# Moving a decay tile, a factor tile and the gate rows from the serial start into the woven first block, with other PSUM banks for the first two state updates

## The reference, cut to what matters

```python
for t in range(S):                                   # layer 1, per head
    m_new = maximum(f[t] + m, i[t])
    f_stab, i_stab = exp(f[t] + m - m_new), exp(i[t] - m_new)
    C = f_stab * C + i_stab * outer(v[t], k[t]);  n = f_stab * n + i_stab * k[t]
    y[t] = sigmoid(o[t]) * (C @ q[t]) / maximum(abs(n @ q[t]), 1.0)
x = (sigmoid(x @ w_gate) * (x @ w_val)) @ w_out      # layer 2
xn = x / sqrt(mean(x * x) + 1e-6) * rms_g            # layer 3
out = (silu(xn @ w_gate2) * (xn @ w_val2)) @ w_out2
```

## Time and profile before

| | us |
|---|---|
| median of 3 runs | 479.87 (479.75 to 481.87) |
| the profiled execution | 479.75 |
| its span | 478.0 |
| PE busy | 471.9 |
| DVE, ACT, POOL busy | 235.6, 196.1, 102.8 |

### The profile page before, as it was taken

The page is one execution under the profiler, slowest core; times in us unless marked ns, Lnnn a source line. Parts: engine busy times, 40 slices in busy tenths (PEclk is TensorE's granted clock), DMA queues, the critical chain, the costliest instruction groups (busy, mean ns, idle before and its releaser), DMA issues.

```text
span 478.0 us, 9965 instructions
## 1 busy us (share of the span) xinstructions
PE 471.9 (99%) x4115; PEld 455.8 (95%) x4115; DVE 235.6 (49%) x515; ACT 196.1 (41%) x404; POOL 102.8 (22%) x142
## 2 busy tenths in 40 slices
PE   8999999999999999999999999999999999999997
PEld 3899989999999999999999999999999999999997
DVE  8858944562766265435434525560455045504550
ACT  4778346623461636153415744330233023302330
POOL 4989910111111110100004968000000000000000
PEclk9899999999999999999999999999999999999999
DMA  7674610111122011100241520001000100010001
GB/s 259 208 242 136 186 46 29 60 45 45 32 85 60 1 45 57 46 1 1 100 149 31 193 93 1 2 1 39 5 1 2 41 1 3 0 43 1 2 2 41
DMA packets 11475, 27.92 MB, mean 58 GB/s; under 512 B 1526, under 2 KB 5830, under 8 KB 11430
## 3 DMA queue, kind: packets, MB, share of 16 engines
q1 hardware_dynamic: 11110, 27.20, 17.7%
q10 hardware_dynamic: 320, 0.08, 0.1%
HBM read 25.23 MB, written 1.97 MB: 57 GB/s over the span
## 4 chain that ended last, share of the span: by engine, by line
PE 89%; DVE 4%; ACT 2%; POOL 1%; DMA 1%; issue 1%; DVEq 0%; ACTq 0%; POOLq 0%
PE bank L1010 26%; PE bank L961 9%; PE bank L962 9%; PE bank L1030 9%; PE bank L1031 9%; PE bank L1032 8%; PE bank L964 6%; PE bank L909 3%; PE bank L882 2%; PE bank L1040 2%; PE bank L837 2%; PE bank L901 1%; DMA raw_x<-in_w_gv 1%; PE bank L858 1%; PE bank L860 1%
## 5 line engine op out<-in xcount | busy, mean ns | idle before, releaser
L961 PE MATMUL bank<-x_hi,wgv_hi 128*128 128x256 f32 x432 | 121.1, 290 | 0.0
L962 PE MATMUL bank<-x_lo,wgv_hi 128*128 128x256 f32 x432 | 118.0, 283 | 0.0
L585 ACT ACTIVATE sg<-bank 128x256 f32<-128x256 f32 (+1 forms) x120 | 51.2, 427 | 156.5 <-PE bank L962 79.6
L1030 PE MATMUL bank<-wo_hi,h_hi 128*128 128x320 f32 x288 | 90.3, 314 | 0.7 <-DVE h_lo L797 0.7
L792 DVE TENSOR_TENSOR hf<-sg,bank 128x256 f32<-128x256 f32 (+1 forms) x120 | 56.7, 473 | 67.0 <-ACT sg L585 64.1
L1010 PE MATMUL bank<-x_hi,wgv_hi 64*128 64x384 f32 x576 | 89.0, 333 | 0.0
L1031 PE MATMUL bank<-wo_lo,h_hi 128*128 128x320 f32 x288 | 89.0, 309 | 0.0
L1032 PE MATMUL bank<-wo_hi,h_lo 128*128 128x320 f32 x288 | 89.0, 309 | 0.0
L961 PEld LDWEIGHTS bank<-x_hi,wgv_hi 128*128 128x128 f32 x432 | 82.6, 191 | 1.3
L962 PEld LDWEIGHTS bank<-x_lo,wgv_hi 128*128 128x128 f32 x432 | 82.7, 191 | 0.4
L964 PE MATMUL bank<-x_hi,wgv_lo 128*128 128x256 f32 x288 | 81.4, 283 | 0.0
(11 more groups left out here) (116 smaller groups left out, 522.1 us busy)
## 6 DMA issues: line engine op xcount, KB each, us to landing
step<-in_w_gv SPq DMA_DIRECT2D x7, 576.0 KB, 3.8
step<-in_vok SPq DMA_DIRECT2D x12, 324.0 KB, 3.0
step<-in_qk_t SPq DMA_DIRECT2D x24, 160.0 KB
raw_x<-in_w_gv SPq DMA_DIRECT2D x5, 576.0 KB, 4.8
raw_p<-in_w_gv SPq DMA_DIRECT2D x4, 576.0 KB, 4.9
y<-y_tok SPq DMA_DIRECT2D x12, 160.0 KB, 1.8
step<-in_vok SPq DMA_DIRECT2D x10, 180.0 KB, 3.5
step<-in_q_t SPq DMA_DIRECT2D x10, 180.0 KB, 2.6
```

The costliest lines, as they stand in the source:

```text
L585: act.activation(sg[:, f % 2, 0:w], g_view(lay, n), ACT.Sigmoid).then_inc(sg_done, 1)
L961: pe.matmul(ps, wgv_hi[:, wc, s, cs], x_hi[:, xs, s, :], start=(s == 0), stop=False)
L962: mm = pe.matmul(ps, wgv_hi[:, wc, s, cs], x_lo[:, xs, s, :], start=False, stop=(s == 2))
L1030: pe.matmul(ps, h[0][:, f, ts], wo_hi[:, f, :], start=(f == 0), stop=False)
```

## The change

1. **The table FIRST.** The PE, ACT, POOL and DVE pieces of tile 2 and 3 stand two slots later than before (S2 in slot 3 instead of 1, K2 and N2 in 5 instead of 3, D3 in 7 instead of 5, S3 and T2 in 9 instead of 7, K3 and N3 in 11, Y3 in 12), T3 in 14 instead of 12, F2 in 14 and R2 in 15. D2 and R1 are no longer part of the serial start: they stand in slots 1 and 2. The gate rows of part 2 are spread over slots 4, 10, 12 and 13.
2. **Banks.** The state updates of tiles 0 and 1 go to PSUM banks 7 and 5 instead of 3 and 1. `hidden(0, 1)` no longer waits for `cn_done`; D2 waits for `cn_done` 2 and R1 for `cn_done` 1.
3. **The serial start.** On DVE, the steps 3 and 4 of the rows of part 1 stand behind the tiles' T and K. On POOL, `vk` of tiles 0 and 1 and the split of chunk 0 stand ahead of the `l_row` step of part 1, and the wait for `consts` 3 is gone. On ACT, F1 stands behind the copies of chunks 1 and 2.
4. **d_rhs.** POOL sets all of it (128x2048) to zero ahead of the first `consts`; DVE and ACT then fill 48 rows each instead of 64. `l_row` has 48 rows instead of 64; `half_neg` is set later.

```diff
-FIRST = [[], [("S", 2)], [], [("K", 2), ("N", 2)], [("Y", 2)], [("D", 3)], [], [("S", 3), ("T", 2)], [("A", 2, 0)],
-         [("K", 3), ("N", 3)], [("Y", 3), ("A", 2, 1)], [("A", 2, 2)], [("T", 3), ("A", 2, 3), ("A", 2, 4)], [("F", 2)],
-         [("R", 2)], []]
+FIRST = [[], [("D", 2)], [("R", 1)], [("S", 2)], [("A", 2, 0)], [("K", 2), ("N", 2)], [("Y", 2)], [("D", 3)],
+         [], [("S", 3), ("T", 2)], [("A", 2, 1)], [("K", 3), ("N", 3)], [("Y", 3), ("A", 2, 2)], [("A", 2, 3), ("A", 2, 4)],
+         [("T", 3), ("F", 2)], [("R", 2)]]
...
-            return bank[(3, 1)[n]] if n < 2 else bank[4]
+            return bank[(7, 5)[n]] if n < 2 else bank[4]
...
-            pool.memset(half_neg[:, :], -0.5).then_inc(consts, 1)
+            pool.memset(d_rhs[:, :, :].bitcast(F32), 0.0).then_inc(consts, 1)
...
-            pool.wait_ge(consts, 3)
+            piece(("D", 0))
+            piece(("D", 1))
+            split(0, 0)
...
-            piece(("D", 0))
-            piece(("D", 1))
-            for c in range(4):
+            for c in range(1, 4):
                 split(0, c)
-            piece(("D", 2))
...
-            piece(("F", 1))
             high(0, 1)
             high(0, 2)
+            piece(("F", 1))
             piece(("T", 0))
             piece(("T", 1))
-            piece(("D", 2))
-            piece(("R", 1))
             high(0, 3)
...
-            for sub in range(5):
-                rows(1, sub)
+            rows(1, 0)
+            rows(1, 1)
+            rows(1, 2)
...
             for n in range(B):
                 piece(("T", n))
+            rows(1, 3)
             for n in range(B):
                 piece(("K", n))
+            rows(1, 4)
...
-                        if n > B:
-                            pe.wait_ge(cn_done, min(n, NT - B))
+                        pe.wait_ge(cn_done, min(n, NT - B))
...
-                if n == 1:
-
-                    pe.wait_ge(cn_done, B)
...
-            piece(("D", 2))
-            piece(("R", 1))
```

More of the change, by code:

```diff
@@ L132, in mlstm_moe_kernel @@
         d_lhs = sb("d_lhs", [P, S], F32R)
-        l_row = sb("l_row", [2 * Q, S], F32R)
+        l_row = sb("l_row", [Q + R, S], F32R)
         cst = [sb(f"cst{b}", [KR, HE], F32) for b in range(B)]
@@ L460, in _ @@
                                         pattern=[[D, nh], [0, D1]], channel_multiplier=-1))
+            pool.memset(half_neg[:, :], -0.5)
             pool.memset(eps[:, :], EPS).then_inc(consts, 1)
-            pool.wait_ge(consts, 3)
+            piece(("D", 0))
+            piece(("D", 1))
+            split(0, 0)
             pool.wait_ge(high_done, 2)
@@ L562, in _ @@
             for b in range(B):
-                act.activation(d_rhs[2 * Q:P, H * b:H * b + H, :],
-                               sel[2 * Q:P, b, :].unsqueeze(2).to_broadcast([2 * Q, H, P]),
+                act.activation(d_rhs[2 * Q:3 * Q + R, H * b:H * b + H, :],
+                               sel[2 * Q:3 * Q + R, b, :].unsqueeze(2).to_broadcast([Q + R, H, P]),
                                ACT.Copy).then_inc(selc_done, 1)
@@ L766, in _ @@
             for b in range(B):
-                dve.tensor_tensor(d_rhs[0:2 * Q, H * b:H * b + H, :],
-                                  l_row[:, 0:P].bitcast(F32).unsqueeze(1).to_broadcast([2 * Q, H, P]),
-                                  sel[0:2 * Q, b, :].unsqueeze(2).to_broadcast([2 * Q, H, P]), ALU.mult).then_inc(drhs_done, 1)
-            for sub in range(5):
-                rows(1, sub)
+                dve.tensor_tensor(d_rhs[0:Q + R, H * b:H * b + H, :],
+                                  l_row[:, 0:P].bitcast(F32).unsqueeze(1).to_broadcast([Q + R, H, P]),
+                                  sel[0:Q + R, b, :].unsqueeze(2).to_broadcast([Q + R, H, P]), ALU.mult).then_inc(drhs_done, 1)
+            rows(1, 0)
+            rows(1, 1)
+            rows(1, 2)
             for n in range(B):
@@ L866, in piece @@
                     pe.wait_ge(lend_done, n)
+                    pe.wait_ge(cn_done, 1)
                     if n > 1:
```

## The result

| | before | with the change |
|---|---|---|
| median, us | 479.87 (5 runs, 479.75 to 481.87) | 484.55 (5 runs, 483.95 to 485.38) |
| ratio to before | | 1.0088, 95% interval 1.0064 to 1.011 |
| profiled execution, us | 479.75 | 484.59 |
| its span, us | 478.0 | 482.8 |

The account below looks back on a forecast made before the run. The prediction took PE, busy 471.9 of 478.0 us, as the bound. Its terms, -1.6 - 0.25 + 1.4 + 0.9 = +0.45 on the profiled 479.75, gave 480.2 us, with a range from 478.7 to 482.0.

Parts of the forecast that it names:

- The gaps of slots 12 and 13, -1.6: PE's idle of 0.88 and 0.70 us waiting for DVE in slots 12 and 13 would go: -1.6 us.
- D2 and R1 between the blocks, +1.4: On PE, D2 and R1 leave a gap and stand between hidden blocks, all on the path: +1.4 us.
- The wait at K2, +0.9: PE would wait at K2 until 37.5 us for ACT's chain with four table loads and DVE's weighing: +0.9 us.
- A table switch with a drain: Rival: on ACT, a pause behind each of four table loads ahead of K2, 5.2 us more, 485.4 us; chance 0.01.
- The start, -0.25: PE would start `hidden(0, 0)` at 22.2 us, as DVE's last copy of Y1 ends earlier: -0.25 us.
- The memset of `d_rhs`, hidden: POOL's memset would delay the constants by 1.8 us, covered by 2.9 us before PE's first D: no cost.
- DVE steps 3 and 4 of part 1, nothing won: These steps, 0.6 us, leave a place where DVE then waited for PE: no gain.
- The clock as a rival: Clock falls after idle ahead of `hidden(0, 0)` or at K2; 3.4 us of hidden blocks lose 1.7: 481.9 us; chance 0.13.

Follow-up runs that it names:

- run 7: Kernel before with only Y3 and the rows of part 2 moved behind the last `h_lo`, T3, F2 and R2 later: 478.82 us, ratio 0.9962.
- run 1: Changed kernel with POOL's `l_row` step back ahead of `vk` of tiles 0 and 1 and the split of chunk 0: 480.58 us, ratio 1.0003.
- run 6: Changed kernel with POOL's order of before, no memset of `d_rhs`, and R1 in slot 1 behind D2: 479.39 us, ratio 0.998.
- run 3: Kernel before with only POOL's `vk` of tiles 0 and 1 and split of chunk 0 put ahead of `l_row`: 484.5 us, ratio 1.0059.
- run 4: Changed kernel with nine more matmuls on zeros on PE between S1 and N0: 484.33 us, ratio 1.007.
- run 5: Changed kernel with POOL's order of before and without the memset of `d_rhs`: 481.95 us, ratio 1.0025.

## Why the prediction was wrong, step by step

- **The gaps of slots 12 and 13, -1.6: right.** No idle in the changed kernel; run 7 measured this part alone at -1.8 us (0.9962 of 480.77, with an interval from -0.8 to -2.8), close to the 1.6 of the two waits.
- **D2 and R1 between the blocks, +1.4: right.** D2 took 30.67 to 31.59 us, R1 about 0.4.
- **The wait at K2, +0.9: right** in mechanism and size, 0.84 in the changed kernel and 0.85 in run 1. K2 was forecast 15.3 us behind the first hidden block and came 15.4 behind it. Run 6 showed the cause, the table loads.
- **A table switch with a drain: fell.** The Sigmoid began 0.01 to 0.02 us behind its load each time, as in the earlier trace rows.
- **The start, -0.25: this step failed.** It came out at +4.28. The prediction weighed POOL's new order only for DVE's last copy in Y1, 9 us later, and priced the moved POOL pieces nowhere else. It had the means to see it: POOL idles for 5 us behind the constants before, DVE is busy all that time, and the prediction itself read from the earlier trace rows that a DVE copy took 0.88 beside a POOL step and might end 0.6 earlier without it. It did not ask what DVE does at 10.8 us, where the order let `vk` start. In its place the runs showed this: `vk` and the first split hold up three DVE steps, the weighing starts 1.6 us later, PE idles 2.0 us ahead of N0, and 10.3 us run at the low clock. Run 1 takes the whole loss away with this one part; run 3 brings 0.6% with it alone.
- **The memset of `d_rhs`, hidden: only nearly.** Its 1.8 us was right (2.44 to 4.24), and the first D on PE was not later for it. But the masks of `bdm` now ran until 10.3 us, in the time of DVE's gate rows and fill, which the prediction did not ask about; DVE's fill began 0.28 later, and PE waited 0.3 for `d_rhs` ahead of 8.63 (0.2 in run 6, without the memset and with D at 8.30).
- **"DVE steps 3 and 4 of part 1, nothing won": right**, but they were the only reserve, 0.55 us, against 2.1 us of delay (three steps of 0.52, 0.58 and 0.70, and 0.3 by which the fill of `d_rhs` began later).
- **The clock as a rival** was priced at one more stretch of 3.4 us in the hidden blocks, 1.7 us. It came as 10.3 us in the serial start, where 3.4 had been before. N0 and N1 alone lost 2.9 us by it. With 1.63 for the late N0 this makes 4.6; 0.3 came back, since T1 no longer waited for Y1. The step had the sign right and the place wrong: it looked at idle that the table made, not at idle in the serial start.

How much of the 4.3 us is lateness and how much the clock is told by the profile (1.6 and 2.9) but not by a run of its own: run 4, made for it, moved the low clock instead of taking it away. One comparison on record bears on it: at the same mean clock of 0.989 the changed kernel took 484.0 to 484.6 us and the kernel before 481.8 to 482.3. So some 2.5 us of the loss stay when both have the low clock for equally long, and some 2.2 are what the kernel before itself loses between 0.996 and 0.989. Why the low clock lasts longer in the changed kernel stays open.

## What to carry to other kernels

A wait that seems useless on an engine with nothing to do can keep it out of another engine's way: before a POOL step is let go earlier, read what DVE does at that time, and remember that one profile shows one phase of several. Where two engines disturb each other, add the delay on the one that the next stage waits for, and look whether the idle that it makes on PE comes where the clock can fall. And try the parts of a bundle apart: here the late Y3 alone won 0.4% (run 7), POOL's order alone lost 0.6% (run 3), and the rest cost about what the late Y3 won (run 1, with both: 1.0003).

## What the runs showed of the hardware

- **DVE beside POOL.** A scan of 16 rows went from 0.41 to 0.93 us, a cast of 16x128 from 0.22 to 0.92, each ending just behind a POOL step that it did not depend on. POOL suffers too: a select of 0.31 took 1.17 beside DVE's fill of `d_rhs`. The Trainium skill (SBUF — State Buffer, section "SBUF: two separate sides") has DVE and GpSimd take turns on a shared port pair for whole instructions. By that rule, the trace agrees: the scan was 0.52 longer with 0.66 of POOL's step to go, the step at 12.01 was 0.58 longer with 0.71 to go.
- **The clock.** In the kernel before PE was busy for 6.4 of the 6.5 us from 10 to 16.5, in run 1 for all of 10 to 16.8, and the granted clock still fell to 1.2 GHz there, during matmuls of 41 columns. In the changed kernel it fell at the end of 2.0 us of idle and stayed low for 10.3 us, although PE was busy all through N and K.
- **One program, several times.** The kernel before fell on 479.7, 480.4 to 481.1 or 481.8 to 482.3 us, with 0.996, 0.993 or 0.989 as mean clock. A profile is one of these. Medians of versions can differ by 1 us merely by how often each occurs, as in run 5.
